# A gated expert on TensorE: the low weight part of the last 64 channels on half of the array's rows, and activation columns stored token by token

## What is computed

```python
# x: 4 x 4160 x 192, eight heads; w_in: 192 x 1024; conv_w: 3 x 1024; w_out: 1024 x 192
w = softmax(weight_gen)                            # over the 7 taps of each token and head
x = einsum('bshk,bskhg->bshg', w, windows_of(x))   # each token sees itself and 6 before it
h = maximum(x @ w_in, 0.0)
conv_out = sum(conv_w[k] * hp[:, k:k + S, :] for k in range(3))   # along the tokens
gate = 1.0 / (1.0 + exp(-conv_out))
out = (h * gate) @ w_out
```

## Time and profile before

| | us |
|---|---|
| median of 3 runs | 718.4 (718.36 to 718.78) |
| profiled execution | 718.5 |
| its span, first to last instruction | 716.7 |
| PE busy, share of the span | 99% |
| DVE and POOL busy | 86% each |
| ACT busy | 69% |

### The profile page before, as it was taken

How to read it: one execution, slowest core, us unless ns; L and a number is a source line. 1 busy time by engine, 2 the same in 40 slices (tenths; PEclk the granted TensorE clock), 3 DMA queues, 4 the chain that set the end, 5 groups by cost and what they waited for, 6 DMA issues and landing times.

```text
span 716.7 us, 9863 instructions
## 1 busy us (share of the span) xinstructions
PE 706.4 (99%) x3839; PEld 634.6 (89%) x3839; DVE 614.3 (86%) x549; ACT 497.3 (69%) x636; POOL 614.2 (86%) x285
## 2 busy tenths in 40 slices
PE   8997999999999999999999999999999999999998
PEld 8756889899999999999989898989899999999997
DVE  7998999999988989898898989898999989885630
ACT  3658867696767676776977676677777867676641
POOL 5999999999997999999899999989898899925310
PEclk9999999999999999999999999999999999999999
DMA  8420312103031222212030210203020200000001
GB/s 239 145 104 1 91 51 77 44 22 100 18 100 30 72 60 55 86 36 95 23 101 16 69 50 23 93 23 108 27 93 23 50 21 20 23 18 23 23 29 34
DMA packets 26297, 41.44 MB, mean 58 GB/s; under 512 B 3864, under 2 KB 23678, under 8 KB 24461
## 3 DMA queue, kind: packets, MB, share of 16 engines
q1 hardware_dynamic: 26250, 40.81, 18.7%
HBM read 28.02 MB, written 12.78 MB: 57 GB/s over the span
## 4 chain that ended last, share of the span: by engine, by line
PE 95%; ACT 2%; DVE 2%; issue 0%; DMA 0%; SPq 0%; ACTq 0%
PE out_ps L952 45%; PE z L930 41%; PE turn_ps L974 3%; PE turn_ps L952 2%; PE z L942 1%; PE z L991 1%; PE turn_ps L991 0%; PE out_ps L991 0%; ACT hidden L634 0%; PE z L952 0%; DVE z L773 0%; DVE z L779 0%; ACT gated L653 0%; DMA logits<-in_weight_gen 0%; DVE xb L824 0%
## 5 line engine op out<-in xcount | busy, mean ns | idle before, releaser
L486 POOL TENSOR_TENSOR weighted<-x_win,soft 128x1344 f32<-128x1344 f32 (+1 forms) x128 | 351.1, 2764 | 7.4 <-DMA x_win<-in_x 7.3
L952 PE MATMUL out_ps<-wo,gated 128*128 128x192 f32 x2000 | 346.0, 326 | 0.2
L952 PEld LDWEIGHTS out_ps<-wo,gated 128*128 128x128 f32 x2000 | 326.9, 190 | 8.4 <-ACT out_sb L689 0.8
L603 POOL TENSOR_TENSOR gated<-gated,hidden 128x1022 f32<-128x1022 f32 (+1 forms) x117 | 248.4, 2123 | 73.9 <-ACT gated L653 73.7
L773 DVE SCALAR_TENSOR_TENSOR z<-hidden,cw,z 128x1022 f32<-128x1022 f32 (+1 forms) x134 | 164.6, 1229 | 59.8 <-ACT z L640 59.0
L634 ACT ACTIVATE hidden<-z 128x1024 f32<-128x1024 f32 (+1 forms) x136 | 134.5, 989 | 106.5 <-PE z L930 99.0
L779 DVE SCALAR_TENSOR_TENSOR z<-hidden,cw,z 128x1022 f32<-128x1022 f32 (+1 forms) x134 | 166.2, 1240 | 4.2
L640 ACT ACTIVATE z<-hidden,cw 128x1022 f32<-128x1022 f32 (+1 forms) x134 | 144.9, 1081 | 4.2
L814 DVE TENSOR_REDUCE attn_a<-weighted 128x256 f32<-128x1792 f32 (+1 forms) x62 | 124.8, 2012 | 0.0
L653 ACT ACTIVATE gated<-z 128x1022 f32<-128x1022 f32 (+1 forms) x117 | 115.1, 984 | 12.0 <-PE out_ps L952 7.1
L930 PE MATMUL z<-xa_hi,wa_hi 128*128 128x512 f32 (+1 forms) x264 | 100.1, 458 | 5.4 <-ACT gated L653 5.2
(11 more groups left out here) (83 smaller groups left out, 394.6 us busy)
## 6 DMA issues: line engine op xcount, KB each, us to landing
x_win<-in_x SPq DMA_DIRECT2D x11, 1344.0 KB, 6.4
out<-out_sb SPq DMA_DIRECT2D x111, 96.0 KB
logits<-in_weight_gen SPq DMA_DIRECT2D x12, 224.0 KB
x_win<-in_x SPq DMA_DIRECT2D x2, 1008.0 KB
out<-out_sb SPq DMA_DIRECT2D x16, 84.0 KB
x_win<-in_x SPq DMA_DIRECT2D x1, 1176.0 KB
x_win<-in_x SPq DMA_DIRECT2D x1, 768.0 KB, 10.1
wo<-in_moe_w_out SPq DMA_DIRECT2D x1, 768.0 KB, 13.9
```

Of the source, the lines that this page charges most:

```text
L486: return engine.tensor_tensor(to, rows, s, ALU.mult)
L603: nc.gpsimd.tensor_tensor(gated_flat(c, n), gated_flat(c, n), hidden[:, n % 3, 1:1 + c.size], ALU.mult) \
L952: last = nc.tensor.matmul(bank[0:end - begin, 0:D], gated[:, j, begin:end], wo[:, j, :], start=(j == 0), stop=(j == J - 1))
```

## The change

The columns of `xa_hi`, `xa_lo`, `xb` and `z` now stand token by token: token i of all partitions, then token i + 1. With 128 partitions and 4 tokens in each bank, bank 0 holds tokens 0 to 3 and bank 1 tokens 4 to 7. ACT and DVE write these buffers in plain runs, and the ReLU puts the order right: it reads `z` with a step of one block of columns (`c.parts`, 128) and writes `hidden` in the order of the tokens.

In `xb`, bank 0 keeps high over low; in bank 1 the high part stands on partitions 64 to 127 and the low part on 0 to 63 (`side_of`, `other`). The fourth pass (`wb_hi`) still uses all 128 rows. The fifth (`wb_lo`) uses only the 64 rows of the high part: the upper half of the array for bank 0, the lower half for bank 1. In the last chunk, with one bank, it uses partitions 0 to 63. So the product of the two low parts of these channels is left out.

```diff
         def columns(buffer, c, part):
-            return buffer[:, c.ring, 0:c.cols].rearrange("p (a i) -> p a i", i=c.tokens)[:, :, part]
+            return buffer[:, c.ring, part.start * c.parts:part.stop * c.parts]
+        def side_of(c, part):
+            return slice(D2, P) if c.banks == 2 and part.start >= c.half else slice(0, D2)
+        def other(rows):
+            return slice(0, D2) if rows.start else slice(D2, P)
         def turned(c, r, rows, at, count):
-            return bank_of(c, r)[rows, at * c.parts:(at + count) * c.parts].rearrange("p (i a) -> p a i", a=c.parts)
+            return bank_of(c, r)[rows, at * c.parts:(at + count) * c.parts]
...
-                nc.scalar.activation(hidden[:, n % 3, 0:c.cols].rearrange("p (a b) -> p a b", a=c.banks),
-                                     z[n % 3][:, 0:c.banks, 0:c.cols // c.banks], ACT.Relu).then_inc(s_hidden, 1)
+                tokens = z[n % 3].rearrange("p b w -> p (b w)")[:, 0:c.cols].rearrange("p (i a) -> p a i", a=c.parts)
+                nc.scalar.activation(hidden[:, n % 3, 0:c.cols].rearrange("p (a i) -> p a i", i=c.tokens), tokens, ACT.Relu) \
+                    .then_inc(s_hidden, 1)
...
-                    to = xa_hi if rows == slice(0, P) else xb[0:D2]
+                    to = xa_hi if rows == slice(0, P) else xb[side_of(c, part)]
...
-                        nc.vector.tensor_tensor(columns(xb[D2:P], c, part), src, columns(xb[0:D2], c, part).bitcast(F32),
+                        side = side_of(c, part)
+                        nc.vector.tensor_tensor(columns(xb[other(side)], c, part), src, columns(xb[side], c, part).bitcast(F32),
                                                 ALU.subtract).then_inc(s_lo, 1)
...
-                parts = [(wa_hi[:, f], a_hi), (wa_hi[:, f], a_lo), (wa_lo[:, f], a_hi), (wb_hi[:, f], b), (wb_lo[:, f], b)]
+                parts = [(wa_hi, a_hi), (wa_hi, a_lo), (wa_lo, a_hi), (wb_hi, b), (wb_lo, b)]
...
-                        last = nc.tensor.matmul(z[n % 3][:, bank, 0:width], weights,
-                                                moving[:, bank * width:(bank + 1) * width],
+                        rows = slice(0, P) if m < 4 else side_of(c, slice(bank * c.half, c.tokens))
+                        last = nc.tensor.matmul(z[n % 3][:, bank, 0:width], weights[rows, f],
+                                                moving[rows, bank * width:(bank + 1) * width],
                                                 start=(m == 0), stop=(m == len(parts) - 1))
```

More of the change, by code:

```diff
@@ L109, in local_attention_gated_expert @@
     PA, COLS = FIRST.parts, FIRST.cols
+    assert FIRST.cols == 1024 and all(c.banks == 1 or c.parts * c.half == 512 for c in CHUNKS)
     assert J == 8 and TAPS == 3 and D2 * 2 == P and COLS <= 1024 and LAST.cols <= COLS
```

## The result

The changed kernel takes 738.6 us (median of 4 runs, 738.56 to 740.89) against 718.5 us: 20.1 us more, a ratio of 1.0287 with a 95% interval of 1.0267 to 1.0307. Forecast were 744 us. Its profiled execution took 738.56 us, with a span of 736.7 us.

A forecast was written before the change was run, and what follows sets the result against it. PE, busy 99% of the span and 95% of the chain, was taken as the bound; 718.5 + 24.3 (two-bank steps) + 3.4 (last chunk) - 2 (absorbed) = 744.2, stated as 744 us, range 732 to 761 us holding 82%.

The forecast's parts named there:

- The gain, 29.4 us: Fifth pass on PE: two banks' matmuls overlap, 0.46 us becomes 0.23 us in 128 two-bank steps, saving 29.4 us.
- The second half's load: Fifth pass: the second half's weight load runs beside the first at no extra cost, or follows, adding 0.11 us per step.
- side by side: Fifth pass: both halves' weight loads run together, as do their matmuls, so 0.42 us holds both; forecast 744 us, chance 0.48.
- serial loads: Rival, fifth pass: the second half's load follows the first, 0.11 us more per step, 14.1 us in all; 758 us, chance 0.26.
- no overlap: Rival, fifth pass: the halves' matmuls run one after the other, losing the 29.4 us gain; 774 us, chance 0.08.
- Drain alone: Rival, row changes: loads are done ahead, so only 0.10 + 0.12 us of nothing meets the 0.23 us gain; 718 us, chance 0.05.
- free changes: Rival, fifth pass: fp32r changes its rows at no cost, so PE saves 0.23 us per step; 692 us, chance 0.05.
- Two changes, 0.42 us: Around the fifth pass: going to 64 rows costs 0.20 us and back 0.22 us, gaps plus exposed weight loads.
- The sum of a step, 0.19 us: Two-bank step on PE: 0.46 us becomes 0.23 + 0.42 = 0.65 us, 0.19 us more, 24.3 us over 128 steps.
- Last chunk, 3.4 us: Last chunk's eight steps: one matmul stays one between two changes, adding 8 x 0.42 = 3.4 us.
- Absorbed, 2 us: About ten early steps before 74 us: PE's four waits for ACT absorb some added time, 2 us taken off.
- ReLU, take and low part at nothing: ACT and DVE work: stepped ReLU read costs nothing, take and low part can only get shorter off the path; 0 us.

The follow-up runs named there:

- the run without overlap: Kernel before, with the fifth pass of both banks on rows 0 to 63, so row changes without side-by-side halves: 767.9 us, ratio 1.0697.
- the layout alone: Changed kernel's column order, stepped ReLU read and exchanged parts, but fifth pass on all 128 rows: 718.37 us against 718.37 us for the kernel before.
- the paired orders: Changed kernel with z filled two steps in a row, then two output tiles: 797.2 us with halves (last chunk 128 rows), 803.9 us all on 128 rows.

## Why the prediction was right

**The bound.** PE at 99% and 95% of the chain before, and the same after. A change on PE moved the end by nearly its own size: right.

**The gain, 29.4 us.** Right: 29.3 us, by the run without overlap.

**The second half's load.** The prediction took side by side, with serial loads as the first rival. The starts 3 ns apart decide for side by side. With it fall serial loads (758 us) and no overlap (774 us). The Trainium skill says so too ("TensorEngine Tiling (Array Packing)", section "Key Properties": tiles load weights and multiply in parallel), and the trace agrees. Drain alone (718 us) falls with the exposed loads, and free changes (692 us) with the gaps of 0.10 us.

**Two changes, 0.42 us.** The mechanism was right, the size a little high: 0.40 us. The way to 64 rows is 0.10 + 0.10 us, as read from the two places ahead of the first step. The way back was put at 0.22 us, with 0.12 us of nothing worked out from the small transpose of 24 rows; it measures 0.09 to 0.10 us, and with the load 0.20 us. The reading of that place was off: the small piece was given 0.04 us, as if its load had 24 columns. The row of its load, which was not among the rows, has 128:

```profile
16.97 0.13 PEld L1023 LDWEIGHTS z<-ident,gated 24*128 24x128 f32 x1
```

It is an `nc.tensor.transpose`, like L974. Behind a change the load ahead of such transposes is exposed for 0.06 us and not 0.11 us (46 of the 128 steps), which the prediction had not looked at. With that, and 0.02 us for 24 streamed columns, 0.08 us of the 0.16 us are left for the way back, an estimate that fits the steps.

**The sum of a step, 0.19 us.** This is the term that was mis-sized. By the parts it is 0.87 - 0.70 = 0.17 us before an output tile or a pass and 0.12 us before transposes, (82 x 0.17 + 46 x 0.12) / 128 = 0.15 us, and 0.145 us from start to start. 128 x 0.045 us = 5.8 us of the forecast did not come.

**Last chunk, 3.4 us.** 2.5 us by the run with 128 rows there, as two of the eight steps had a wait to fill.

**Absorbed, 2 us.** The waits of PE for ACT hardly shrank:

```profile
PE z L942 <- ACT gated L663: 5.0, 4, 1.8
```

5.0 us after, 5.2 us before. The likely reason, which no run tests, is that the waits moved along with the work: ACT's chain starts from z, so what PE adds delays its partner as well. Between the starts of the first and the ninth step, 0.7 us were added instead of 1.2 us, and 0.9 us in the next eight: some 0.7 us were absorbed. The parts as measured give 18.6 + 2.5 - 0.7 = 20.4 us, against 20.1 us. Against the forecast, the step was 5.8 us too dear, the last chunk 0.9 us too dear, and 1.3 us too much had been taken off for waits. So the forecast owes little to errors that cancel: it stayed 5 us too high, and the step is nearly all of that.

**ReLU, take and low part at nothing.** Right, by the layout alone.

## What to carry to other kernels

Before putting a small matmul on part of the array's rows, count the changes of row use, not only the slots saved: here one change cost 0.20 us (0.15 us on the way back where transposes follow), nearly as much as a whole matmul of 512 columns (0.23 us). A pair of halves between full-height work saves one slot of 0.23 us, pays 0.40 us and loses. By the same numbers two pairs in a row would save 0.46 us and win a little; no run shows such a win. A cost of this kind can often be read before the change is made, in a corner of the same trace: two short stretches in the first 29 us showed gap and exposed load to within 0.03 us. And a reordering that halves a cost must be checked against every shared buffer behind it, the output bank as well as the input ring.

## What was not expected of the hardware

- Behind a change, the load ahead of an `nc.tensor.transpose` was exposed for 0.06 us, half of the 0.10 to 0.11 us before other matmuls; the 128 columns are the same. The matmuls of L991, which multiply by the identity without being such transposes, belong to the others: the first two behind the change at 17.14 us start 0.21 us apart instead of 0.11 us.
- A ReLU that reads PSUM with a step of 128 columns over two banks takes 1025 ns for 1024 elements, no more than a plain one.
- In the paired orders, with PE waiting often, the mean granted clock of the profiled executions was 0.987 and 0.981; in all other kernels every execution had 0.995 or more.
